# Attention, gated feed-forward and routed experts in one kernel: a reordered first norm, pairs of groups from group 20, and turned sums

## The reference

```
attn = softmax(masked q k^T / 8) v            # 4 batches, 8 heads, 576 tokens, head size 64
                                              # heads 0-3: the last 32 keys; heads 4-7: keys of the same residue mod 32
x    = attn as [2304 tokens, 512]
xn   = x / sqrt(mean(x*x) + 1e-6) * rms_g     # "the norm"
g    = xn @ w_gate;  val = xn @ w_val         # 512 -> 1536
y    = (silu(g) * val) @ w_out                # 1536 -> 512
out  = gate_w * (relu(y @ w1[e]) @ w2[e])     # e = the best of 8 experts for each token
```

## Time and profile before

| | |
|---|---|
| median of 3 runs | 863.51 us (862.11 to 865.79) |
| the profiled execution | 865.16 us, span in the trace 863.4 us |
| PE busy | 847.0 us, 98% of the span |
| DVE, ACT, POOL busy | 535.7, 369.6, 330.5 us (62%, 43%, 38%) |
| mean granted clock of PE | 0.994 of full speed |
| share of PE in the chain that ended last | 86% (DVE 7%, POOL 2%, ACT 1%) |

### The profile page before, as it was taken

How to read it: one execution, slowest core, us unless ns; L and a number is a source line. 1 busy time by engine, 2 the same in 40 slices (tenths; PEclk the granted TensorE clock), 3 DMA queues, 4 the chain that set the end, 5 groups by cost and what they waited for, 6 DMA issues and landing times.

```text
span 863.4 us, 15547 instructions
## 1 busy us (share of the span) xinstructions
PE 847.0 (98%) x5203; PEld 732.6 (85%) x5203; DVE 535.7 (62%) x1400; ACT 369.6 (43%) x934; POOL 330.5 (38%) x373
## 2 busy tenths in 40 slices
PE   9999999999999999999999999999999999999996
PEld 5678898999889998999999998987888888888885
DVE  6975565444563446548788764884887457666663
ACT  6966414445354355443221132243456235554441
POOL 3735772434432633544346333070043122222212
PEclk9989999999999999999999999999999999999999
DMA  8974212312132210242131121626275645555531
GB/s 193 283 176 125 60 45 65 96 57 80 51 101 61 65 38 25 74 159 74 37 98 61 61 74 37 226 67 257 98 239 186 232 146 194 200 202 193 194 118 40
DMA packets 77517, 103.40 MB, mean 120 GB/s; under 512 B 38973, under 2 KB 43069, under 8 KB 77312
## 3 DMA queue, kind: packets, MB, share of 16 engines
q1 hardware_dynamic: 73760, 91.16, 33.5%
q0 software_dynamic: 3680, 11.28, 3.8%
HBM read 92.98 MB, written 10.22 MB: 120 GB/s over the span
## 4 chain that ended last, share of the span: by engine, by line
PE 86%; DVE 7%; issue 3%; POOL 2%; ACT 1%; DVEq 0%; POOLq 0%; ACTq 0%
PE ps L1251 31%; PE ps L1290 15%; PE ps L1855 13%; PE ps L1840 13%; PE ps L1176 3%; PE ps L1211 2%; PE ps L1865 2%; PE ps L1190 2%; PE ps L1150 2%; PE ps L1332 1%; PE ps L670 1%; DVE h L1641 1%; POOL sm L1046 1%; DVE h_lo L1646 1%; DVE w_lo L2094 1%
## 5 line engine op out<-in xcount | busy, mean ns | idle before, releaser
L1046 POOL TENSOR_TENSOR sm<-sm,rinv 72x288 f32<-72x288 f32 (+1 forms) x51 | 45.6, 893 | 168.8 <-DVE rinv L1577 168.8
L1078 POOL TENSOR_TENSOR out_lo<-out_raw,out_hi 128x512 fp32r<-128x512 f32 x72 | 101.8, 1414 | 5.8
L1076 POOL CAST out_hi<-out_raw 128x512 fp32r<-128x512 f32 x72 | 52.6, 730 | 132.9 <-DMA out_raw<-in_moe_w_out 132.9
L1251 PE MATMUL ps<-x_hi,gate_hi 128*128 128x384 f32 x288 | 100.1, 348 | 0.6 <-DVE h L1635 0.6
L1635 DVE SCALAR_TENSOR_TENSOR h<-h,ps 128x384 f32<-128x384 f32 x72 | 39.8, 552 | 97.4 <-ACT h L1469 96.5
L1251 PE MATMUL ps<-x_hi,val_hi 128*128 128x384 f32 x288 | 98.5, 342 | 0.0
L1251 PE MATMUL ps<-x_hi,gate_lo 128*128 128x384 f32 x288 | 96.9, 337 | 0.0
L1251 PE MATMUL ps<-x_hi,val_lo 128*128 128x384 f32 x288 | 96.4, 335 | 0.0
L1251 PE MATMUL ps<-x_lo,val_hi 128*128 128x384 f32 x288 | 96.3, 334 | 0.0
L1251 PE MATMUL ps<-x_lo,gate_hi 128*128 128x384 f32 x288 | 93.7, 335 | 0.0
L1290 PE MATMUL ps<-out_hi,h_hi 128*128 128x512 f32 x216 | 88.4, 409 | 1.3 <-DVE h_lo L1646 1.3
(11 more groups left out here) (288 smaller groups left out, 1937.8 us busy)
## 6 DMA issues: line engine op xcount, KB each, us to landing
w_raw<-in_moe_w SPq DMA_DIRECT2D x72, 512.0 KB, 4.4
out_raw<-in_moe_w_out SPq DMA_DIRECT2D x72, 256.0 KB, 2.6
x_rows<-y_tiles SPq DMA_DIRECT2D x18, 256.0 KB, 2.8
early_w_raw<-in_moe_w SPq DMA_DIRECT2D x8, 512.0 KB, 4.3
gate_raw<-in_moe_w_gate SPq DMA_DIRECT2D x4, 768.0 KB, 8.3
val_raw<-in_moe_w_val SPq DMA_DIRECT2D x4, 768.0 KB, 10.0
qk<-in_q SPq DMA_DIRECT2D x8, 288.0 KB
qk<-in_k SPq DMA_DIRECT2D x8, 288.0 KB
```

What stands on the lines that cost most here:

```text
L1046: pool.tensor_tensor(s3, s3, rinv[0:n, i, :].unsqueeze(2).to_broadcast([n, 4, c]), ALU.mult).then_inc(s_no, 1)
L1076: pool.tensor_copy(oh[i][:, :], o_raw[i][:, :]).then_inc(s_oh, 1)
L1078: pool.tensor_tensor(ol[i][:, :], o_raw[i][:, :], oh[i][:, :].bitcast(f32), ALU.subtract).then_inc(s_ol, 1)
L1251: mm = pe.matmul(ps[:, bank, 0:CH], w[:, i, kk, cols], x[:, kk, :], start=(m == 0), stop=(m == n - 1))
```

## The change

Five edits go together.

- **The first norm.** The mean's factor moves into a column `share` of 1/512, so the sums come out as a mean. The sum over the first three head pairs goes to one bank, the last pair's squares to another, and DVE adds them. The third step of the inverse root's iteration is folded into the second, with a factor 3/8 that moves into `rms_gain`: seven short steps in place of nine behind the first guess, and the guess takes one step in place of two. The spread is three transposes of a broadcast column in place of a product of ones with diagonal tiles. The spread stands ahead of the turn of group 15, the dummies are placed anew (44 in the head before and now), and x is split on ACT ahead of its group work of that tick.
- **Groups 14 to 19.** The values product of 14 and 15, and all later steps of 16 to 19, go behind the first products. The first feed-forward step is written as four blocks, `first_block`: gate high (8 matmuls), value high (8), gate low (4), value low (4).
- **Pairs from group 20** where it was 28. Groups 20 to 27 are scored at ticks 3, 8, 22 and 34 behind `EARLY`, turned at 13, 20, 32 and 44. All later pairs are scored four ticks sooner in the six-tick pattern.
- **Turned sums** in chunks 1 to 5: the squares are transposed (three of 128 columns) and added up by DVE, where three columns were made with six passes of a product with ones.
- The split of the first quarter of `w_val` goes from tick 13 to 11, and the last squares of chunk 0 from tick 16 to 15.

The core of the diff:

```diff
@@ tables
-    return EARLY + SPAN - 6 + 12 * ((j - 2 * NG) // 2)
+    return EARLY + SPAN - 10 + 12 * ((j - 2 * NG) // 2)
...
-PAIRS = 2 * NG
+PAIRS = HEAD
-TURN.update({HEAD - 3 + i: EARLY + 1 + 2 * i for i in range(3)})
-PV = {j: TURN[j] + (1 if j < HEAD - 1 else 2) for j in range(G)}
+SCORE[HEAD - 1] = EARLY + 1
+TURN.update({HEAD - 4 + i: EARLY + 3 + 2 * i for i in range(4)})
+TURN.update({HEAD + i: EARLY + (13, 20, 32, 44)[i // 2] for i in range(2 * NG - HEAD)})
+PV = {j: TURN[j] + (1 if j < HEAD else 2) for j in range(G)}
+PV.update({HEAD - 6: EARLY + 1, HEAD - 5: EARLY + 2})
...
-SPLIT_V = {0: 13, 1: at(0, 1, 1), 2: at(0, 4, 1), 3: at(0, 7, 1)}
+SPLIT_V = {0: 11, 1: at(0, 1, 1), 2: at(0, 4, 1), 3: at(0, 7, 1)}
@@ front_pe
+            def sum_squares(of, bank, done=s_ssq):
+                for t in range(TT):
+                    mm = pe.matmul(ps[:, bank, t:t + 1], of[:, t * P:(t + 1) * P], share[:, :],
+                                   start=True, stop=True)
+                mm.then_inc(done, 1)
...
+            def turn_squares(c):
+                bank_7_free(("ss", c))
                 pe.wait_ge(s_sq, sq_steps(c + 1))
                 for t in range(TT):
                     cols = slice(t * P, (t + 1) * P)
-                    mm = pe.matmul(ps[:, ss_bank(c), t:t + 1], nr[:, cols], ones[:, 0:1], start=True, stop=c > 0)
...
+                    mm = pe.transpose(ps[:, ss_bank(c), cols], nr[:, cols], ident[:, :])
                 mm.then_inc(s_ssq, 1)
             def spread_roots(c):
-                pe.wait_ge(s_dg, c + 1)
-                pe.matmul(ps[:, rb_bank(c), 0:CH], ones[:, :], diag[:, :, :].rearrange("p t n -> p (t n)"),
-                          start=True, stop=True).then_inc(s_rb, 1)
+                pe.wait_ge(s_nw, 8 * c + 8)
+                for t in range(TT):
+                    mm = pe.transpose(ps[:, rb_bank(c), t * P:(t + 1) * P], root[:, t:t + 1].to_broadcast([P, P]),
+                                      ident[:, :])
+                mm.then_inc(s_rb, 1)
...
                 if s == SS[0] + 1:
-                    sum_squares(0)
+                    first_sums()
+                    pe.wait_ge(s_qe, TURNED_QK[EARLY])
+                    pe.wait_ge(s_sq, sq_steps(1))
+                    sum_squares(sq, rb_bank(0))
+                    keep_busy(2)
+                if s == SPREAD[0]:
+                    keep_busy(2)
+                    spread_roots(0)
...
-                    if sub == 0:
+                    if s < EARLY + 4:
+                        first_block(sub, half)
+                    elif sub == 0:
@@ front_dve, roots
-                link(dve.tensor_scalar(halved[:, :], var[:, :].bitcast(i32), 1, None, ALU.logical_shift_right))
...
-                dve.tensor_tensor(diag[:, :, :], ident[:, :].unsqueeze(1).to_broadcast([P, TT, P]),
-                                  root[:, :].unsqueeze(2).to_broadcast([P, TT, P]), ALU.mult).then_inc(s_dg, 1)
```

More of the change, by code:

```diff
@@ L1049, in square @@
             def square(c, kk):
-                first = max(i for i, (hp, g) in enumerate(GROUPS) if hp == kk and not (c == 0 and hp < 2 and g == 2))
+                first = max(i for i, (hp, g) in enumerate(GROUPS) if hp == kk and (hp > 1 or 2 * LQ * g <= (CH * c + CH - 1) % S))
                 pool.wait_ge(s_oe, NG * last_batch(c) + first + 1)
@@ L1081, in front_pool @@
             for s in range(TICKS):
+                for j in NORM_AT.get(s, []):
+                    normalise(j)
                 if s < EARLY:
@@ L1254, in product, with first_block @@
                     mm.then_inc(done, 1)
+            def first_block(low, val):
+                if not low:
+                    if val:
+                        pe.wait_ge(s_oe, VALUED[EARLY - 1])
+                        pe.wait_ge(s_wl, 4)
+                    else:
+                        pe.wait_ge(s_qe, TURNED_QK[EARLY])
+                        pe.wait_ge(s_wl, 2)
+                wh, wl = (vh, vl) if val else (gh, gl)
+                for kk in range(KT):
+                    for w, x in ((wh, xl),) if low else ((wh, xh), (wl, xh)):
+                        if not val:
+                            pe.wait_ge(s_xl if low else s_xh, kk + 1)
+                        mm = pe.matmul(ps[:, val, 0:CH], w[:, 0, kk, 0:P], x[:, kk, :],
+                                       start=(low == 0 and kk == 0 and w is wh), stop=(low == 1 and kk == KT - 1))
+                if low:
+                    mm.then_inc(s_vp if val else s_g, 1)
             def gate_product(c, f, half):
                 if half == 0:
-                    if c == 0 and f == 0:
-                        pe.wait_ge(s_qe, TURNED_QK[EARLY])
                     if c == 0 and f % QF == 0:
@@ L1433, in evac_o_pair @@
                 act.wait_ge(s_pv, j + 2)
-                if j % NG == 0:
+                if b >= 2 and j % NG == 0:
                     act.wait_ge(s_xl, KT * b)
@@ L1501, in front_act @@
                     evac_y(c - 1)
[L1502 removed]
+                if (sub, half) == (1, int(s < EARLY + 6)):
                     tanh(FT * c + f)
+                if s == SPREAD[0] + 1:
+                    x_split(0)
                 for j in TURN_AT.get(s, []):
@@ L1603, in roots @@
[L1603 to L1608, removed]
@@ new lines, in roots @@
+                link(dve.tensor_scalar(root[:, :].bitcast(i32), var[:, :].bitcast(i32), -0.5, 1597463007.0,
+                                       ALU.mult, ALU.add))
+                link(dve.scalar_tensor_tensor(out=newt[:, :], in0=root[:, :], scalar=-0.5, in1=root[:, :],
+                                              op0=ALU.mult, op1=ALU.mult))
+                link(dve.tensor_tensor(newt[:, :], newt[:, :], var[:, :], ALU.mult))
+                link(dve.scalar_tensor_tensor(out=root[:, :], in0=newt[:, :], scalar=1.5, in1=root[:, :],
+                                              op0=ALU.add, op1=ALU.mult))
@@ new lines, in roots @@
+                link(dve.tensor_tensor(newt[:, :], root[:, :], root[:, :], ALU.mult))
+                link(dve.tensor_tensor(newt[:, :], newt[:, :], var[:, :], ALU.mult))
+                link(dve.scalar_tensor_tensor(out=newt[:, :], in0=newt[:, :], scalar=-10.0 / 3.0, in1=newt[:, :],
+                                              op0=ALU.add, op1=ALU.mult))
+                link(dve.scalar_tensor_tensor(out=root[:, :], in0=newt[:, :], scalar=5.0, in1=root[:, :],
+                                              op0=ALU.add, op1=ALU.mult))
@@ L1686, in front_dve @@
                     h_split(FT * c + f)
+                if s == SPREAD[0] + 1:
+                    for kk in range(KT):
+                        normalise_x(0, kk)
+                    for j in INVERT_AT[s]:
+                        invert(j)
                 if s < EARLY:
-                    for key in NORMED_AT.get(s, []):
-                        normalise_x(*key)
                     for key in QK_AT.get(s, []):
@@ L1701, in front_dve @@
                         normalise_x(*key)
+                if s == SS[0] + 1:
+                    dve.wait_ge(s_ssp, 1)
+                    dve.tensor_scalar(newt[:, :], ps[:, ss_bank(0), 0:TT], 1e-6, None, ALU.add).then_inc(s_part, 1)
+                for x in SS_AT.get(s - 1, []):
+                    roots(x)
                 if s == SPREAD[0] + 1:
                     x_split(0)
[L1704 to L1707, removed]
+                else:
+                    for j in INVERT_AT.get(s, []):
+                        invert(j)
                 for key in DOT_AT.get(s, []):
```

88 lines of the change are left out of this document (49 added, 39 removed).

## The result

| | before | changed |
|---|---|---|
| median of 14 runs each | 863.62 us (862.11 to 867.44) | 860.25 us (859.32 to 860.86) |
| span of the profiled execution | 863.4 us | 858.8 us |
| PE busy in it | 847.0 us | 841.8 us |
| mean granted clock | 0.994 | 0.997 |

The ratio is 0.9956, with a 95% interval of 0.9943 to 0.9968. The change gains 3.4 us where 9.0 were forecast. The interval excludes no change, so it is faster, but by a little less than the 0.5% that I called measurable. The time lies just inside the wide range of 848.5 to 860.5, and outside the forecast's own of 851 to 857.5; the size of the gain does not hold.

A forecast was written before the change was run, and what follows sets the result against it. PE's queue plus a few short waits was taken to bound the kernel. Terms -0.2 - 2.3 - 2.5 - 4.0 gave -9.0 us, so 863.5 - 9.0 = 854.5 us; range 848.5 to 860.5, the forecast's own 851 to 857.5.

The forecast's parts named there:

- Later chunks, -2.5 and -4.0: Chunks 1 to 5: transposed sums and spread save 2.5 us; scoring later pairs four ticks sooner saves 4.0 us.
- the first two causes: Waits in later chunks: pair inverse behind `roots`, 1.3 us; score beside turning at a chunk's start, 2.1 us; both would end.
- the third cause, `h_lo` (-0.6): Last down product of a chunk waits for `h_lo`, 1.3 us in three times; half was expected to go, -0.6 us.
- First norm, the two starts: First gate product would move from 55.82 to 50.2 us at full clock, or 53.0 if the clock falls again.
- The evacuation waits, +1.2: Groups 16 and 17 in bank 7: turnings and products wait for each other's copies, +1.2 us, bounds 0 and 2.
- the ring: Not forecast, found in the trace: group 21's mask, h, ACT's h_hi and group 17's copy wait in turn, holding PE 3.7 us.
- the first norm's full-clock sum: First norm and block if the clock stays full: -2.1 us; with the half-clock case +1.7, the middle -0.2 was taken.
- Pairs, -2.3: Chunk 0, pairs from group 20: four pairs save 2.1 us, the merged turning of q and k 0.2 more.
- The head before the sums, 0 with 1 to either side: Moving the `w_val` split two ticks forward ends waits at ticks 15 and 16, may make them at 13 and 14.
- The new wait: Rival: eighteen pairs wait 0.25 us each on normalisation, losing 4.5 us of gain, time 859; chance 0.15.
- the slower rival: Clock stays at half from 47.3 us through the first block until about 80 us, time 868; chance 0.04.
- my own signs of being wrong: PE's waits in chunks 0 to 3 sum to as much as before, or the half clock lasts beyond 60 us.

The follow-up runs named there:

- both mends: Changed kernel with ACT's queue reordered, the first w_out split four ticks later and an own probability buffer for group 21: 854.36 us, ratio 0.9904.
- the run with a buffer of its own: Changed kernel with a separate probability buffer for group 21, so its mask need not wait for the turning of group 17: 857.11 us.

## Why the prediction was wrong

- **What bounds the kernel.** Right in the main: where PE waited less or worked less, the time followed. The exception is the end of the program, which scatters by 1.6 us over the profiles with no edit there.
- **Later chunks, -2.5 and -4.0.** Right in sum: -7.2 in the trace, 6.1 by the run with these edits alone. The sooner pairs gave 3.6 by two runs, against 3.4 for the first two causes. On the third cause, `h_lo` (-0.6), the runs differ: with the sooner pairs alone it waited 1.6 us instead of 1.3, with the norm's edits beside them 0.8 (the changed kernel) and 0.7. The sums gave 1.6 in all. The spread was not tried alone. What is left for it and the rest is 0.9 us by the medians, and 2.3 by the trace between matmuls 241 and 1440, where the pieces give 1.6 (0.33 for 0.65, five times).
- **First norm, the two starts.** The start at full clock was right (50.81 for 50.2). The baseline was wrong: the 55.82 of the earlier trace rows holds a half clock that other executions of the same head do not have. At full clock that head starts the product at 52.54 or 53.47 in two profiles, so the reordering wins 1.7 to 2.7 us and not 5. That the profiled execution lay 1.65 us above the median was a sign of this, and I carried it along as a constant.
- **The evacuation waits, +1.2: the step that failed.** "The nearest row is the wait on ACT's copy of a pair, 0.8 us. Nothing is the lower bound, 2 us the upper." I looked at the copy alone and not at what is queued ahead of it on ACT, nor at what that waits for. It is the ring above: 3.7 + 0.4 us of waiting, and a half clock from 64.8 to some 68.2 us behind it. The stretch from the first gate product to matmul 241 shows the size: 1.2 us more had been forecast for it (0.4 + 1.9 + 1.2 - 2.3). It takes 87.65 us, against 81.66 and 81.26 in the two profiles of the old order at full clock, so 6 us more. With both mends it takes 82.85. Opening the ring with the other waits of the block is worth 5.1 us (855.20) and both mends 5.9 (854.36). The 5.1 holds some 0.8 us of POOL beside DVE, which I had not foreseen either.
- **The sum again.** With 5.1 in place of 1.2 for this term, and the first norm's full-clock sum taken from 52.54 (-2.1 + 3.3 = +1.2 in place of -0.2), the sum is -9.0 + 3.9 + 1.4 = -3.7 us. That it comes near the -3.4 measured is in part luck. It is a sum for a kernel before at full clock, and against its runs at a mean clock of 0.998 or more (862.5) the changed kernel gains 2.3. The 1.4 us between the two are not accounted for; 0.8 us can lie in the end of the program, which scatters by more than that.
- **Pairs, -2.3.** Not tried alone. In the changed kernel a pair in chunk 0 costs 1.13 + 0.86 + 0.61 us from start to start, the price that was used. A single wait on POOL of 0.5 us shows, ahead of a turning at 118.9 us.
- **The head before the sums, 0 with 1 to either side.** The sums start at 45.14 us in place of 44.96, inside the bounds.
- **Rivals.** The new wait came, but as one of 3.7 us and not spread over eighteen pairs. The clock did fall behind it, as the slower rival had it, but it was back after 3.4 us, and after 6.8 in the profiles of two experiments. Both of my own signs of being wrong came with it: a half clock beyond 60 us, and waits of PE between 50 and 430 us that sum to 5.6 us, where they had summed to 5.1. The prediction's sentence from the Trainium skill on transposes ("TensorE: Matmul & The Clock Gate", "Part 4: PE-mode transpose") would have made the half clock at the norm likelier. With three transposes in place of the wide product, the clock stayed full through the norm in all nine profiles with the changed head. That does not show that transposes count, only that here it cost nothing.

## What to carry to other kernels

When a step is moved, write down for each engine what stands ahead of it in that engine's queue and what that waits for, and follow it until it comes back to the step itself; a buffer's former user is part of the path. The order of a few queue entries was worth 5.1 us here, and the new arithmetic of five norms 2.5 by the medians (6.1 less 3.6). Check whether a half clock in the profiled execution is the kernel's or that execution's before counting on its end.

## What the runs showed of the hardware

- An idle stretch of PE of 3.7 us, with little work ahead of it, was followed by 1.2 GHz for about 3.4 us (64.8 to 68.2) in the changed kernel. Two profiles with the same wait had 6.8 us at 1.2 GHz. With a single wait of 1.7 us (the run with a buffer of its own) the clock fell all the same, at 63.9 us for 3.4; with waits of 1.2 and 1.8 us apart it stayed at 2.4 GHz in one profile. The length of the wait alone does not sort these.
- The same instructions of the head ran once with a clock of 0.50 for 6.8 us and twice at 1.00. Run by run, the kernel before took 862.5 us on average at a mean clock of 0.998 or more and 864.9 below. What decides between the two was not tested.
- Three transposes of 128 columns take 0.33 us in PE's stream, and the nine wide products behind them take 2.09 us, as much as behind other work (2.08). The product over diagonal tiles took 0.65.
- DVE's four `x_lo` took 4.51 us beside four elementwise instructions on POOL, 2.85 beside two, and 1.96 beside none.
